# Fused attention and feed-forward kernel: probabilities turned in half-height blocks, scores copied negated out of PSUM, engines re-ordered

## The reference

```python
q_rot, k_rot = (rotate(q), rotate(k))
scores = scale * np.matmul(q_rot, k_rot.transpose(0, 1, 3, 2))
scores = scores - np.max(scores, axis=-1, keepdims=True)
attn = np.exp(scores)
attn = attn / (np.sum(attn, axis=-1, keepdims=True) + 1e-09)
attn_out = np.matmul(attn, v)
...
h = x @ w_in
g = np.maximum(h, 0.0) + alpha * np.minimum(h, 0.0)
out = g @ w_out
```

## Time and profile before

| what | value |
|---|---|
| median of 3 runs | 698.59 us (695.95 to 699.34) |
| the profiled execution's own time | 699.36 us |
| its span, first to last instruction | 697.6 us |
| PE busy | 683.6 us, 98% of the span |
| DVE, ACT, POOL busy | 370.2, 316.9, 269.2 us |
| PE's share of the chain that ended last | 94% |
| start of tile 0 in periods 0, 1 and 2 | 13.55, 28.18, 52.31 us |
| first transposes of the 17th period | 283.09 us |

### The profile page before, as it was taken

How to read it: one execution, slowest core, us unless ns; L and a number is a source line. 1 busy time by engine, 2 the same in 40 slices (tenths; PEclk the granted TensorE clock), 3 DMA queues, 4 the chain that set the end, 5 groups by cost and what they waited for, 6 DMA issues and landing times.

```text
span 697.6 us, 12233 instructions
## 1 busy us (share of the span) xinstructions
PE 683.6 (98%) x4152; PEld 594.0 (85%) x4152; DVE 370.2 (53%) x682; ACT 316.9 (45%) x746; POOL 269.2 (39%) x258
## 2 busy tenths in 40 slices
PE   7889999999999999999999999999999999999998
PEld 7758888888888887698889999999999999999996
DVE  4758888888888887645643333234223422333322
ACT  2747777777777776533333222322222232223223
POOL 5565577667776512222222222222222222222222
PEclk9989999999999999999999999999999999999999
DMA  6896766655566644600001000100000000001001
GB/s 157 192 233 148 180 151 138 150 135 133 133 137 146 146 112 125 242 0 1 1 0 46 1 1 5 41 1 0 15 30 0 0 30 15 0 1 45 1 2 45
DMA packets 76879, 51.30 MB, mean 74 GB/s; under 512 B 61348, under 2 KB 61732, under 8 KB 76324
## 3 DMA queue, kind: packets, MB, share of 16 engines
q1 hardware_dynamic: 76402, 50.26, 28.7%
q10 hardware_dynamic: 434, 0.49, 0.3%
HBM read 22.95 MB, written 4.72 MB: 40 GB/s over the span
## 4 chain that ended last, share of the span: by engine, by line
PE 94%; SPq 2%; DMA 1%; DVE 1%; POOL 1%; ACT 0%; issue 0%
PE banks L667 29%; PE banks L696 28%; PE banks L587 13%; PE banks L545 11%; PE banks L609 10%; PE banks L605 2%; DMA k_two<-k_hi 1%; DMA raw_k<-in_k 0%; DMA cos_sb<-in_cos 0%; SPq L322 0%; DVE nmax L922 0%; SPq L304 0%; DVE pt L971 0%; SPq L321 0%; POOL swapped L412 0%
## 5 line engine op out<-in xcount | busy, mean ns | idle before, releaser
L482 POOL TENSOR_TENSOR g_lo<-g,g_hi 128x384 fp32r<-128x384 f32 (+1 forms) x98 | 99.8, 1018 | 309.6 <-ACT g_hi L867 306.4
L1037 DVE TENSOR_SCALAR g<-banks,alpha_sb 128x384 f32<-128x384 f32 (+1 forms) x98 | 59.8, 610 | 250.9 <-ACT pos L858 250.9
L667 PE MATMUL banks<-x_hi,w_in_lo 128*128 128x384 f32 x384 | 129.3, 337 | 0.0
L667 PE MATMUL banks<-x_hi,w_in_hi 128*128 128x384 f32 x384 | 129.2, 337 | 0.0
L667 PE MATMUL banks<-x_lo,w_in_hi 128*128 128x384 f32 x384 | 129.0, 336 | 0.0
L858 ACT ACTIVATE pos<-banks 128x384 f32<-128x384 f32 x96 | 47.1, 491 | 170.3 <-PE banks L667 170.3
L922 DVE TENSOR_REDUCE nmax<-banks 128x1 f32<-128x576 f32 x144 | 108.7, 755 | 27.4 <-PE banks L545 21.7
L696 PE MATMUL banks<-w_out_hi,g_hi 128*128 128x512 f32 x288 | 114.8, 399 | 0.3
L696 PE MATMUL banks<-w_out_hi,g_lo 128*128 128x512 f32 x288 | 112.9, 392 | 0.0
L696 PE MATMUL banks<-w_out_lo,g_hi 128*128 128x512 f32 x288 | 111.9, 389 | 0.0
L867 ACT ACTIVATE g_hi<-g 128x384 fp32r<-128x384 f32 (+1 forms) x98 | 50.9, 519 | 116.0 <-DVE g L1040 116.0
(11 more groups left out here) (86 smaller groups left out, 905.9 us busy)
## 6 DMA issues: line engine op xcount, KB each, us to landing
k_two<-k_hi SPq DMA_DIRECT2D x62, 160.0 KB, 2.9
out<-stage SPq DMA_DIRECT2D x18, 256.0 KB, 2.0
raw_q<-in_q SPq DMA_DIRECT2D x32, 128.0 KB, 2.7
raw_k<-in_k SPq DMA_DIRECT2D x32, 128.0 KB, 2.4
q_two<-q_hi SPq DMA_DIRECT2D x32, 128.0 KB, 2.3
q_two<-q_lo SPq DMA_DIRECT2D x32, 128.0 KB, 2.4
q_own<-q_hi SPq DMA_DIRECT2D x32, 128.0 KB, 2.4
raw_v<-in_v SPq DMA_DIRECT2D x32, 128.0 KB, 2.3
```

Of the source, the lines that this page charges most:

```text
L482: nc.gpsimd.tensor_tensor(g_lo[f % 2][:, part], g[f % 2][:, part], g_hi[f % 2][:, part].bitcast(F32), ALU.subtract).then_inc(g_lo_done, 1)
L667: mm = nc.tensor.matmul(h_ps[f % 2], w[:, j, cols], xx[:, j, :], start=(step == 0), stop=(step == 3 * CT - 1))
L1037: nc.vector.tensor_scalar(g[f % 2][:, part], h_ps[f % 2][:, part], 0.0, alpha_sb[:, f:f + 1], ALU.min, ALU.mult).then_inc(neg_done, 1)
```

## The change

Four things are changed, and the order of three engines with them.

1. `turn_two` replaces `turn` for the units of `prob`: two units together, each 128x128 block as two transposes of 64 rows, rows 0 to 63 into one bank and rows 64 to 127 into the next. A pair of units is 16 transposes of 64x128 instead of 8 of 128x128. `flat` then copies a bank that holds one half of the rows of both units (`pt_half`).
2. `maxima` is now a `tensor_scalar` that multiplies the PSUM tile by -1, writes it to `prob` and gives its minimum as `nmax`; `exps` works in place on `prob` with scale -1. `score` waits for `maxima`, not for `exps`. The waits on `turned` for the reuse of `prob` move from ACT to DVE.
3. Of the flat copies of a period, three (`U_PB[3]`, `U_PA[0]`, `U_PA[2]`) move from DVE to ACT; `U_MIXED` comes before `U_K`; the sum's 1e-9 is added by a `tensor_tensor`.
4. On SP, in period 0, k's load for pair 2 goes out ahead of the stack of pair 1 and of the values. The values' loads have a semaphore for each buffer.

```diff
-U_Q, U_K, U_MIXED = 7, 8, 9
+U_Q, U_MIXED, U_K = 7, 8, 9
...
+    def pt_half(par, u):
+
+        head, units = (0, U_PA) if u in U_PA else (1, U_PB)
+        two, half = divmod(units.index(u), 2)
+        slot = pt_slot(par, head, two * 2)
+        return pt[:, slot:slot + 2, 0:QT * P].rearrange("p w (i r c) -> p r w i c", r=2, c=REM)[:, half, :, :, :]
...
-                    if has_pair(p + 2) and not is_opening(p):
+                    if has_pair(p + 2):
                         load(p + 2, 1)
                     if has_pair(p + 1):
                         stack(p + 1, (t + 1) % 2, 0)
                         stack(p + 1, (t + 1) % 2, 1)
                     if is_opening(p):
                         load_v(b, t)
-                        load(p + 2, 1)
...
                 if not (isinstance(s, int) and s < 2):
-                    pe.wait_ge(exp_done, s - 1)
+                    pe.wait_ge(max_done, s - 1)
...
+            def turn_two(p, t, u):
+
+                if not exists_now(p, u):
+                    return
+                halves = (fill(p, u), fill(p, u + 1))
+                if u in U_PA:
+                    pe.wait_ge(exp_done, p * TILES + (1 + QT))
+                    first = U_PA.index(u) * P
+                else:
+                    first = S + REM + U_PB.index(u) * P
+                pe.sem_inc(pair_filled, 1)
+                for w in range(2):
+                    for i in range(QT):
+                        for bank, r in zip(halves, (slice(0, D), slice(D, P))):
+                            to = (w * QT + i) * D
+                            mm = nc.tensor.transpose(bank[:, to:to + D], prob[r, i, first + w * P:first + (w + 1) * P],
+                                                     ident[r, r])
+                mm.then_inc(turned, 2)
...
                 turn(p, t, U_KREM)
+                turn_two(p, t, U_PB[0])
                 score(p, t, A_TILES[0])
-                turn(p, t, U_PB[0])
-                turn(p, t, U_PB[1])
-                turn(p, t, U_PB[2])
                 score(p, t, A_TILES[1])
-                turn(p, t, U_PB[3])
+                turn_two(p, t, U_PB[2])
                 turn(p, t, U_Q)
...
-                turn(p, t, U_PA[0])
-                turn(p, t, U_PA[1])
-                turn(p, t, U_PA[2])
+                turn_two(p, t, U_PA[0])
                 score(p, t, B_TILES[2])
-                turn(p, t, U_PA[3])
                 score(p, t, B_TILES[3])
-                pv(p, par, 1)
+                turn_two(p, t, U_PA[2])
+                pv(b, t, 1)
...
-                nc.scalar.activation(dst.rearrange("p (h s) -> p h s", h=2), s_ps[(t * TILES + n) % 2],
-                                     ACT.Exp, bias=nmax[:, t % 2, n:n + 1],
+                nc.scalar.activation(row_of(n), row_of(n), ACT.Exp, scale=-1.0, bias=nmax[:, t % 2, n:n + 1],
                                      accum_out=rsum[:, t % 2, n:n + 1]).then_inc(exp_done, 1)
...
-                nc.vector.tensor_reduce(nmax[:, t % 2, n:n + 1], s_ps[(t * TILES + n) % 2], AX.XY,
-                                        ALU.max, negate=True).then_inc(max_done, 1)
+                nc.vector.tensor_scalar(row_of(n), s_ps[(t * TILES + n) % 2], -1.0, None, ALU.mult, ALU.min,
+                                        accum_out=nmax[:, t % 2, n:n + 1]).then_inc(max_done, 1)
...
-                    nc.vector.tensor_scalar(rsum[:, par, :], rsum[:, par, :], 1e-9, None,
+                    nc.vector.tensor_tensor(rsum[:, par, :], rsum[:, par, :], tiny[:, :].to_broadcast([P, TILES]),
                                             ALU.add).then_inc(sum_done, 1)
```

More of the change, by code:

```diff
@@ L29 @@
 OF_NEXT = (U_Q, U_K)
+OF_NEW = (U_Q, U_MIXED, U_K)
 def build(nc, q, k, v, w_in, w_out, alpha, cos, sin, eye, out):
@@ L103, in build, with half_bank, row_of @@
     PT_REM = 3 * QT
+    def pt_half(par, u):
[3 more added lines that the diff above has]
+        return pt[:, slot:slot + 2, 0:QT * P].rearrange("p w (i r c) -> p r w i c", r=2, c=REM)[:, half, :, :, :]
+    def half_bank(bank):
+        return bank.rearrange("p (w i c) -> p w i c", w=2, c=REM)
+    def row_of(n):
+        if n == REM_TILE:
+            row = prob_rem[:, 0:S]
+        else:
+            head, i = divmod(n - 1, QT)
+            row = prob[:, i, head * S:(head + 1) * S]
+        return row.rearrange("p (h s) -> p h s", h=2)
     def both_ends(keys):
@@ L415, in rope @@
                         ALU.mult).then_inc(rope_step, 9 if first and a == 0 else 1)
-                pool.wait_ge(turned, unit_count(p - 2, U_MIXED))
+                pool.wait_ge(turned, unit_count(p - 2, U_K if side else U_MIXED))
                 nc.gpsimd.tensor_tensor(
@@ L553, in turn @@
                 bank = fill(p, u)
-                if u in U_PA:
-                    pe.wait_ge(exp_done, p * TILES + (1 + QT))
-                    blocks = [prob[:, i, U_PA.index(u) * P:(U_PA.index(u) + 1) * P] for i in range(QT)]
-                elif u in U_PB:
-                    first = S + REM + U_PB.index(u) * P
-                    blocks = [prob[:, i, first:first + P] for i in range(QT)]
-                elif u == U_KREM:
+                if u == U_KREM:
                     pe.wait_ge(exp_done, p * TILES)
@@ L792, in flat @@
                     jobs = [(pt[r, PT_REM, QT * P:S], bank[r, r]) for r in HEADS]
-                elif u in U_PB:
-                    jobs = [(pt[:, pt_slot(t % 2, 1, U_PB.index(u)), 0:QT * P], bank)]
-                elif u in U_PA:
-                    jobs = [(pt[:, pt_slot(t % 2, 0, U_PA.index(u)), 0:QT * P], bank)]
+                elif u in U_PB or u in U_PA:
+                    jobs = [(pt_half(t % 2, u), half_bank(bank))]
                 else:
@@ L961, in flat @@
                 bank = t_ps[u % T_BANKS]
-                if u in U_PB:
-                    jobs = [(pt[:, pt_slot(t % 2, 1, U_PB.index(u)), 0:QT * P], bank)]
-                elif u in U_PA:
-                    jobs = [(pt[:, pt_slot(t % 2, 0, U_PA.index(u)), 0:QT * P], bank)]
+                if u in U_PB or u in U_PA:
+                    jobs = [(pt_half(t % 2, u), half_bank(bank))]
                 elif u == U_QREM:
@@ L1070, in period @@
                         split_x(0, 0, j)
-                if not is_opening(p):
-                    maxima(p, t, B_TILES[0])
+                maxima(p, t, B_TILES[0])
                 maxima(p, t, B_TILES[1])
-                flat(p, U_PA[0], t)
+                if is_opening(p):
+                    lo(p, U_K, t)
                 normalise(p, *before, 0)
@@ L1080, in period @@
                 maxima(p, t, B_TILES[2])
-                flat(p, U_PA[2], t)
                 maxima(p, t, B_TILES[3])
```

111 lines of the change are left out of this document (56 added, 55 removed).

## The result

The changed kernel takes 692.82 us (691.27 to 695.99, 6 runs) where the kernel before took 697.56 in the same comparison (695.58 to 699.34, 6 runs): ratio 0.9935, interval 0.9913 to 0.9957. It is faster by 4.7 us. The forecast was 686.2, a gain of 12.4 us, so less than half of the forecast gain came.

A forecast was written before the change was run, and what follows sets the result against it. PE, busy 98% of the span, was taken as the bound. 7.60 (wait) + 0.3 (opening) + 15 x 0.30 (periods) = 12.4 off 699.36 gives 687.0, median 686.2; range 678 to 698, the forecast's own 683 to 691.

The forecast's parts named there:

- The wait in period 1: Period 1: with k's load early, PE's wait for rot_k and the slow clock go, 7.60 us back.
- The opening: Period 1's start: half blocks done inside the wait for a stack; 0.3 us gained, bounds 1.2 gained to 0.7 lost.
- the k load is hidden, the rest of the opening gains 0.3 net: Opening: k's early load fits SP's free 1.34 us; 0.81 us of work done earlier, less 0.5 for late stacks.
- the wait for bank 0: Copies of U_PB[0], U_PA[1] and U_KQREM behind ACT's exponentials: first to be late if PE's time fails to cover them.
- The half blocks: Each later period: 32 pairs at 0.057 us, side by side, replace 3.49 us of transposes; period 16.23 us, 0.30 less.
- changes of tile: Each later period: entering and leaving four groups of half blocks costs PE 1.365 us; bounds half of it and all.
- The first: Rival: small instructions start too slowly or load and stream partly add; pair 0.082 us, median 698.2, no change; 8%.
- the second rival: Halves are done one after the other; pair 0.11 us, period 1.39 us worse, median 711.6, slower; 9%.
- the fourth: Rival: tile changes cost half of 1.365 us; 10.2 us less, 676; 5%.
- Waits in the later periods: Rival: PE waits for a bank, nmax or a stack, half a microsecond a period; 693.7 us; 10%.
- The step on DVE's operation: DVE's `tensor_scalar` with a minimum, not in the trace: taken as 0.8 us, between 754 ns and 0.92.

The follow-up runs named there:

- the load alone: Kernel before with only k's load for pair 2 moved ahead of stack and values in period 0 (values' semaphore for each buffer): 693.59 us, ratio 0.9939.
- the run with the queue shortened: Kernel before, k's load for pair 2 early but issued by ScalarE, values of pair 1 behind the stacks of pair 2: 692.62 us, ratio 0.992.
- fillers: Changed kernel plus eight 128x128 identity multiplications, results never read, in the 17th period only: 691.17 us, ratio 0.9907.
- the last version: Changed kernel with full-height single-bank transposes in the 17th period and period 0, and SyncE's queue shortened in periods 0 and 1: 690.10 us, ratio 0.9887.

## Why the prediction was right and wrong

In the profile 5.7 us came of the 12.4 forecast. The 6.7 that are missing are 3.6 in the 17th period, 1.6 in the opening, 1.3 in periods 2 to 15 and 0.2 in the rest. The median, 692.82, lies above the forecast's own range (683 to 691, where its terms give only 683.9 to 689.6). It is inside 678 to 698, but that range had been widened for waits in the later periods, which did not come: that it holds is luck.

**The wait in period 1: right.** 24.13 us became 17.17 with no wait for rot_k and a clock of 1.00, and the load alone gives that part of the gain. POOL goes on at once from q to k (26.32 us) and is done at 30.3, as forecast (30.2).

**The opening: wrong, by 1.6 us.** The step "the k load is hidden, the rest of the opening gains 0.3 net" failed. Taken to tile 0 of period 2, 6.57 us came for a forecast of 8.2. Tile 0 of period 1 starts 0.39 us later than before, and period 1 takes 17.17 us where 16.23 was forecast, with a wait of 0.64 for an exponential (30.25). With the 0.3 that were to be gained, these make the 1.6. Period 0 itself grew by 1.29 us (14.63 to 15.92), but 0.90 of it is only the earlier start of tile 0, given back at the stack. The wait for k_lo ahead of the first pair of half blocks is 1.46 us for 0.43. k_lo is ready 2.05 us after k's transposes start (22.22), as before (2.08 us after 21.49), but only 0.6 us of PE's work stands between them, for 1.65. A pair, which needs two banks, can't start in that time; with one bank at a time four transposes do, and the wait is 0.98. The last two copies of period 0 stand behind one another on ACT, and with two of the four copies back on DVE and single banks the waits of 0.58 and 0.64 fall to 0.17 and 0.22. The prediction had named the wait for bank 0 as what is late first if the cover fails, and given it no price in the opening. SP's queue is the next limit, not this one: the changed kernel has no wait for a stack in periods 1 and 2. It shows where PE is earlier, with the load alone (1.12 and 1.25 us, and the run with the queue shortened gets these back) and with period 0 at full height (0.36 and 0.65).

**The half blocks: mechanism right, size off.** The pair costs 0.062 us and not 0.057; that was the upper end of its own range. 16.23 + 32 x 0.005 = 16.39, measured 16.35. With 1.37 us of changes of tile, the gain of a period was a difference of two larger numbers, and 0.005 us in a pair took more than half of it. The first and the second rival are refuted by the same row: a pair takes neither 0.082 nor 0.11. Changes of tile were not half price, which refutes the fourth. That the halves overlap is shown, for one after the other they would take the 0.109 of a whole block. What sets the 0.062 is not shown: in the 17th the starts follow each other evenly, 25 to 36 ns apart, at the same 0.062 for a pair, so a least distance of instructions would fit as well as the streams.

**Waits in the later periods: none**, as forecast. ACT and DVE fit (13.80 us for a forecast of 14.4, and 12.16 for 12.2). The step on DVE's operation was right within 0.04 us (0.754 + 0.083 for 0.8).

**The 17th period: wrong, by 3.6 us.** It stands in no term of the sum, so it was costed at nothing, and no reason was given. But it has no score tiles: nothing covers the copies, and the rule "two banks at once" makes each group wait. The waits cost 1.7 us (8.59 with full blocks in pairs against 6.93 with single banks). The shorter half blocks save 0.7 (4.44 against 5.15 up to `inv`). The half clock then costs 2.5 in the profiled execution: from `inv` to the feed-forward's first matmul it is 5.96 us, against 3.44 with full blocks at a clock of 1.00. A typical execution loses less, for the median with fillers is only 1.6 below.

What stays open: why the opening's gain of the last version (1.3 us in the profile) shows only in part in its median; which of the small waits in the opening cost the clock in single executions; and why the clock falls behind half blocks more often than behind full ones, of which only the height is shown, as odds.

## What to carry to other kernels

Price a change in the periods that are not typical, the first and the last, apart from the steady one: here the steady periods gave 2.9 us and the two ends decided the rest. A unit that takes two buffers at once needs other work beside it; where a pipeline drains, go back to one buffer at a time. A transfer moved ahead in a full queue is not free: name what stands last in that queue. And moving it to another engine's queue helps only where it does not travel with the first loads.

## What the hardware showed that was not expected

- TensorE's granted clock fell to half behind waits of which none was over 0.8 us (0.31 and 0.73, and within the next, of 0.69, in the profiled execution of the changed kernel), when half blocks stood between them, mostly not when full ones did; with eight fillers it was 1.00 in the profiled 17th.
- Two transposes of 64 rows in the two halves of the array start within 9 ns of each other in the later periods, and pairs follow at 0.062 us; their weight loads, 0.138 us each in the trace, do not show.
- `tensor_scalar` with an accumulated minimum is two operations on DVE, of 754 and 83 ns.
